# Fewer filler matmuls between the first scores and the first rows: 5 in place of 24

## The chip, the cores and the metric

The kernel runs on one core of one Trainium2 chip. Its time is the device time of one execution in microseconds (us), lower is better. Times in the trace count from the first instruction of the profiled execution.

## The reference, cut to what matters

Three stages follow one another: a blockwise decayed linear attention, a Fourier mixing with a layer norm and a two-layer network, and a second layer norm with another network. The change touches the attention stage only.

```python
def _attn_ref(q, k, v, lam):                 # B, H, S, D = 2, 8, 768, 64
    ...
    for b in range(nb):                      # blocks of tokens
        intra = np.einsum('bhic,bhjc->bhij', qb, kb) * Dmask[None]
        intra = np.einsum('bhij,bhjd->bhid', intra, vb)
        inter = np.einsum('bhid,bhde->bhie', qb * lam_pow[None], kv_state)
        out[:, :, sl] = intra + inter
        kb_dec = kb * rev_pow[None]
        kv_state = lam_block * kv_state + np.einsum('bhsd,bhse->bhde', kb_dec, vb)
    return out

def reference(**kwargs):
    attn_out = _attn_ref(**attn_kwargs)
    x = ...                                  # (2, 768, 512)
    x = _moe_ref(x=x, **moe_kwargs)          # x + Re(FFT2(x)), norm, 512 -> 2048 -> 512
    return _moe2_ref(x=x, **moe2_kwargs)     # norm, 512 -> 2048 -> 512
```

## The kernel before, in words

Every engine has a program of its own, written out by hand, and semaphores tie them together; there is no scheduler. The order of the work on an engine is the order in its program.

The attention stage works in NBLK = 6 blocks of 128 tokens and B = 2 batches, which gives 12 units (block c, batch b). TensorE has three kinds of steps for a unit, all on f32 data:

- **scores** (`scores_of`, line 374): keys times queries, 8 products, each of 64 rows of the array and 128 columns moved. The product for the even head of a pair lies on partitions 0 to 63, that for the odd head on 64 to 127.
- **keys-values** (`keys_values`, line 387): the block's addition to the state, 8 products with outputs of 64 partitions each. It waits for kd, GpSimd's product of line 1314.
- **rows** (`rows`, lines 404 and 409): masked scores times values (line 409, 8 products of 64 columns), and from block 1 on queries times state (line 404, 4 products of 128 columns). It waits for the masks of VectorE (line 924) and, from block 1, for qd (GpSimd, line 1303) and the state.

An f32 product appears as two instructions in the trace, so a full rows step is 8 instructions of line 404 and 16 of line 409, and a scores step is 16 of line 374.

At the start the order on TensorE is: a wait for the first zeroed state tile (GpSimd, line 1289); 11 filler matmuls (line 417, WARM_BEFORE); scores(0, 0) and scores(0, 1); 24 filler matmuls (line 422, WARM_BETWEEN); a wait for the first values (v_first); rows(0, 0), keys-values(0, 0), rows(0, 1), scores(1, 0), keys-values(0, 1). A loop over blocks 1 to 4 follows, in each of which stand scores(c, 1), keys-values(c, 0), rows(c, 0), scores(c+1, 0), keys-values(c, 1), rows(c, 1). At the end come scores(5, 1), rows(5, 0) and rows(5, 1). A filler matmul multiplies a 128x128 f16 tile of zeros by 128x512 zeros into bank 7, which nobody reads; the bank is later the keys-values output of batch 1, written with start=True.

The masks need the decay matrix DT. VectorE makes the powers of lam (line 908), SyncE writes them to pow_dram (line 274) and reads them back as DT (line 278); the copy of line 913 and the first masks (line 924) wait for that. SyncE's queue loads blocks c = 2 to 5 into two alternating buffers: queries and keys (line 261) wait for qk_done and qd_done, keys and values by token (line 264) for pv_done and kv_done, which TensorE counts up. Weight chunks (line 243) are loaded in between.

Behind the attention stage TensorE goes on with the Fourier products `sequence` (line 472), then `features` (line 491), and for the rest of the kernel with the networks (lines 552 and 572). ScalarE copies each rows result out (line 680), and VectorE (lines 956, 957, 985, 986) and GpSimd (lines 1325, 1326) fold these for the Fourier products.

Of the kernel before, what the change touches and what calls it, by code (L numbers as in the profile page):

```python
# [60 lines left out]
S1, S2, S3, S4, A12, A11, A22 = range(7)  # L61
B11, T1, B21, B22, T3, T2, T4 = X_ORDER = range(7)

WARM_BEFORE, WARM_BETWEEN = 11, 24
LATE = {2: 4, 3: 5}


# [1443 lines left out]
```

## Time and profile before

| | us |
|---|---|
| median of 3 executions | 622.82 |
| lowest, highest | 621.06, 626.46 |
| the profiled execution's own time | 626.46 |
| its span, first to last instruction | 624.5 |

The profile is of one execution. PE is TensorE's matmuls, PEld its weight loads, DVE VectorE, ACT ScalarE, POOL GpSimd, SPq SyncE's DMA queue. The ends of matmuls are modelled, so neighbouring groups overlap by some tenths of a us; where lengths are added up, the distance from one start to the next is used. "Granted clock" is the share of TensorE's full 2.4 GHz that the chip let through: 1.00 is 2.4 GHz, 0.50 is 1.2 GHz.

### The profile page before, as it was taken

The numbers are of one execution on the slowest core, as the hardware profiler recorded it, in microseconds if no ns is written. First come the engines' busy times: TensorE is split into PE (matmuls) and PEld (weight loads), VectorE is DVE, ScalarE is ACT, GpSimd is POOL, SyncE is SP. The second block draws the span as 40 slices with busy tenths as digits, with TensorE's granted clock in tenths as the row PEclk, the third lists the DMA queues.
The fourth block names the chain that finished last, engine by engine and source line by source line (L and its number), as shares of the span: only waits on it lengthen the run. The fifth ranks groups of instructions, "written<-read, shape, count | busy, mean of one in ns | idle before, by whom it ended". The sixth has DMA issues, their size and how long they took to land.

```text
span 624.5 us, 10866 instructions
## 1 busy us (share of the span) xinstructions
PE 597.9 (96%) x4143; PEld 407.7 (65%) x4143; DVE 371.2 (59%) x637; ACT 242.4 (39%) x488; POOL 152.7 (24%) x133
## 2 busy tenths in 40 slices
PE   8999899978989999999999999999999999999997
PEld 4898656745666666666666666576666666666664
DVE  2569948967678586556676888733345334433223
ACT  0332143643465432443356675234422344232231
POOL 1547644833532000110322763001000010000000
PEclk9999699979999999999999999999999999999999
DMA  8999780000000263331123231100001000010001
GB/s 243 392 382 382 274 243 1 1 2 1 0 2 1 76 162 102 101 102 44 60 68 99 71 116 54 34 2 1 1 26 44 1 2 1 0 68 1 1 2 68
DMA packets 41412, 50.43 MB, mean 81 GB/s; under 512 B 2442, under 2 KB 28690, under 8 KB 39956
## 3 DMA queue, kind: packets, MB, share of 16 engines
q1 hardware_dynamic: 39156, 45.05, 21.9%
q10 hardware_dynamic: 1728, 3.15, 1.3%
q0 software_dynamic: 480, 1.57, 0.9%
q8 instruction: 32, 0.52, 0.3%
q14 instruction: 16, 0.13, 0.1%
HBM read 43.46 MB, written 6.30 MB: 80 GB/s over the span
## 4 chain that ended last, share of the span: by engine, by line
PE 66%; DVE 11%; POOL 7%; issue 7%; DMA 5%; ACT 3%; SPq 1%; DVEq 0%; ACTq 0%; POOLq 0%
PE bank L572 30%; PE bank L552 26%; PE bank L472 4%; DMA arena<-attn 3%; PE bank L409 2%; DMA arena<-w 1%; PE bank L404 1%; DVE arena L1034 1%; PE bank L541 1%; POOL arena L1410 1%; DVE arena L1042 1%; DVE arena L1035 1%; DVE arena L1155 1%; POOL arena L1357 1%; POOL arena L1354 1%
## 5 line engine op out<-in xcount | busy, mean ns | idle before, releaser
L572 PE MATMUL bank<-arena 128*128 128x512 f16 x1152 | 288.2, 380 | 2.9 <-DVE arena L1163 2.0
L552 PE MATMUL bank<-arena 128*128 128x256 f16 x2016 | 262.6, 275 | 9.6 <-DVE arena L1204 6.7
L552 PEld LDWEIGHTS bank<-arena 128*128 128x128 f16 x2016 | 198.2, 99 | 85.0 <-DVE arena L1204 7.6
L572 PEld LDWEIGHTS bank<-arena 128*128 128x128 f16 x1152 | 112.7, 98 | 90.2 <-DVE arena L1163 2.6
L1155 DVE SCALAR_TENSOR_TENSOR arena<-arena 128x512 f16<-128x512 f32 x96 | 71.1, 741 | 76.4 <-ACT arena L804 76.3
L804 ACT ACTIVATE arena<-arena 128x512 f16<-128x512 f32 x96 | 60.4, 629 | 101.0 <-DVE arena L1204 95.6
L1198 DVE SCALAR_TENSOR_TENSOR arena<-bank,arena 128x256 f32<-128x256 f32 x48 | 20.2, 422 | 71.8 <-PE bank L552 71.8
L1367 POOL TENSOR_TENSOR arena<-arena 128x512 f32<-128x512 f32 x6 | 8.3, 1379 | 150.9 <-ACT arena L775 90.8
L1149 DVE TENSOR_TENSOR arena<-arena 128x512 f16<-128x512 f32 x42 | 35.5, 855 | 12.2 <-ACT arena L788 12.2
L859 ACT ACTIVATE arena<-bank 128x256 f32<-128x256 f32 x48 | 18.3, 382 | 58.2 <-PE bank L552 58.2
L968 DVE TENSOR_REDUCE arena<-arena 128x1 f32<-128x1024 f32 x32 | 38.3, 1209 | 0.0
L1204 DVE SCALAR_TENSOR_TENSOR arena<-bank,arena 128x256 f32<-128x256 f32 x48 | 20.2, 420 | 27.1 <-PE bank L552 27.1
L472 PE MATMUL bank<-arena 128*128 128x385 f32 (+1 forms) x96 | 34.3, 514 | 0.0
L822 ACT ACTIVATE arena<-bank 128x256 f32<-128x256 f32 x48 | 18.4, 383 | 40.2 <-PE bank L552 40.1
L1182 DVE SCALAR_TENSOR_TENSOR arena<-bank,arena 128x256 f32<-128x256 f32 x48 | 20.2, 421 | 20.2 <-PE bank L552 20.2
L1354 POOL TENSOR_TENSOR arena<-arena 128x256 f32<-128x256 f32 x16 | 14.6, 910 | 69.8 <-DMA arena<-w 65.5
L836 ACT ACTIVATE arena<-bank 128x256 f32<-128x256 f32 x48 | 18.3, 382 | 29.1 <-PE bank L552 29.1
L815 ACT ACTIVATE arena<-bank 128x256 f32<-128x256 f32 x48 | 18.1, 377 | 27.5 <-PE bank L552 27.5
L409 PE MATMUL bank<-arena 128*128 128x64 f32 x192 | 27.8, 275 | 0.7 <-DVE arena L924 0.7
L409 PEld LDWEIGHTS bank<-arena 128*128 128x128 f32 x192 | 26.6, 204 | 1.2 <-issue 1.2
L472 PEld LDWEIGHTS bank<-arena 128*128 128x128 f32 x96 | 18.9, 201 | 12.9 <-issue 2.3
L788 ACT ACTIVATE arena<-arena 128x512 f16<-128x512 f32 x42 | 26.1, 624 | 1.5 <-POOL arena L1374 1.3
(97 smaller groups left out, 556.7 us busy)
## 6 DMA issues: line engine op xcount, KB each, us to landing
arena<-w SPq DMA_DIRECT2D x48, 256.0 KB, 4.5
arena<-w SPq DMA_DIRECT2D x24, 512.0 KB, 3.8
arena<-attn SPq DMA_DIRECT2D x10, 1024.0 KB, 8.8
x_dram<-arena ACTq DMA_DIRECT2D x12, 256.0 KB, 6.5
out<-arena SPq DMA_DIRECT2D x12, 256.0 KB, 2.1
arena<-attn SPq DMA_DIRECT2D x4, 512.0 KB, 4.3
arena<-c SPq DMA_DIRECT2D x1, 1153.5 KB, 11.0
arena<-g SPq DMA_DIRECT2D x1, 514.0 KB, 12.6
```

The source lines that it names most:

```text
L409: last = nc.tensor.matmul(xps[b][:, h * D:(h + 1) * D], PT[b][:, par, pair, :], v, start=first, stop=True, skip_group_check=not first)
L472: last = nc.tensor.matmul(f1_bank[f % 3][:, 0:n], lhs, C1[:, c, par * NE:par * NE + n], start=c == 0, stop=c == HALF - 1)
L552: last = nc.tensor.matmul(bank_, wst[:, i, wx, w, kt, :], xs[s % 2][:, ux, x, kt, :], start=not started and k == 0, stop=k == 5, skip_grou ...
L572: last = nc.tensor.matmul(ops[t][:], hT[n % 2][:, half, hx, t * P:(t + 1) * P], wdn[:, i, wx, half * DM:(half + 1) * DM], start=first and ...
L788: nc.scalar.activation(xs[s % 2][:, 0, which, :, :], x_block(which), ACT.Copy).then_inc(xh_done, 1)
L804: nc.scalar.activation(hT[n % 2][:, half, 0, :], z[n % 2][:, half, :], ACT.Relu).then_inc(hh_done, 1)
L968: nc.vector.tensor_reduce(wmax_chunks[:, m, c:c + 1], raw, AX.X, ALU.max, apply_absolute_value=True).then_inc(wred[m], 1)
L1149: nc.vector.tensor_tensor(xs[s % 2][:, 1, which, :, :], x_block(which), xs[s % 2][:, 0, which, :, :], ALU.subtract).then_inc(xl_done, 1)
L1155: nc.vector.scalar_tensor_tensor(hT[n % 2][:, half, 1, :], z[n % 2][:, half, :], 0.0, hT[n % 2][:, half, 0, :], ALU.max, ALU.subtract).the ...
L1182: nc.vector.scalar_tensor_tensor(z[n % 2][:, 0, 0:HT], chain[1 - n % 2], H_SCALE, p1, ALU.mult, ALU.add).then_inc(z11_out, 1)
L1198: nc.vector.scalar_tensor_tensor(z[n % 2][:, 1, 0:HT], seventh[:, 0:HT], H_SCALE, u2, ALU.mult, ALU.add).then_inc(z21_out, 1)
L1354: nc.gpsimd.tensor_tensor(s1, a21, a22, ALU.add).then_inc(ws_step, 1)
```

## The change

The constant WARM_BETWEEN goes from 24 to 5; nothing else changes. The loop of lines 421 and 422 then issues 5 filler matmuls.

```diff
-WARM_BEFORE, WARM_BETWEEN = 11, 24
+WARM_BEFORE, WARM_BETWEEN = 11, 5
```

## Rows read from the trace of the kernel before

**Rows 1.** The page: granted clock in 40 slices of 15.6 us; the chain's shares.

```profile
PEclk9999699979999999999999999999999999999999
...
PE 66%; DVE 11%; POOL 7%; issue 7%; DMA 5%; ACT 3%; SPq 1%; DVEq 0%; ACTq 0%; POOLq 0%
```

**Rows 2.** Timeline of TensorE: start, length, line, count, idle time before and its releaser.

```profile
7.47 5.35 PE L422 MATMUL bank<-arena 128*128 128x512 f16 x24
13.53 1.97 PE L409 MATMUL bank<-arena 128*128 128x64 f32 x16 [0.71 <-DVE arena L924]
16.03 0.69 PE L387 MATMUL bank<-arena 128*64 128x64 f32 x16 [0.52 <-POOL arena L1314]
16.64 2.00 PE L409 MATMUL bank<-arena 128*128 128x64 f32 x16
18.57 1.16 PE L374 MATMUL bank<-arena 64*128 64x128 f32 x16
...
22.15 0.69 PE L387 MATMUL bank<-arena 128*64 128x64 f32 x16 [0.71 <-POOL arena L1314]
...
25.58 1.16 PE L374 MATMUL bank<-arena 64*128 64x128 f32 x16
26.68 0.69 PE L387 MATMUL bank<-arena 128*64 128x64 f32 x16
27.29 0.49 PE L404 MATMUL bank<-arena 128*128 128x128 f32 x2
...
30.11 1.16 PE L374 MATMUL bank<-arena 64*128 64x128 f32 x16
```

**Rows 3.** Timeline of VectorE, around the first masks, and the fold of one unit.

```profile
11.96 0.24 DVE L913 COPY arena<-arena 128x4 f32<-128x4 f32 x2 [8.06 <-DMA arena<-pow_dram]
12.10 2.48 DVE L924 TENSOR_TENSOR arena<-bank,arena 128x512 f32<-128x512 f32 x4
...
60.79 1.46 DVE L956 TENSOR_TENSOR arena<-arena 128x512 f32<-128x512 f32 x1
62.17 1.75 DVE L957 TENSOR_TENSOR arena<-arena 128x512 f32<-128x512 f32 x1
```

**Rows 4.** The chain that ended last, in order of time: start, length, what.

```profile
9.81 7.68 DMA arena<-attn
...
17.63 2.35 POOL arena L1303
...
22.15 0.69 PE bank L387 x16
```

**Rows 5.** Busy time by stretch; after POOL: the granted clock, DMA share, GB/s.

```profile
63.50:65.70 2.20, 0.05 (x1) 0.00 (x0) 2.20 (x4) 0.60 (x1) 2.20 (x2) 1.00 1.05 404
65.70:71.50 5.80, 5.11 (x24) 5.14 (x25) 5.25 (x6) 0.00 (x0) 2.28 (x2) 0.50 0.57 214
71.50:75.90 4.40, 4.40 (x9) 2.50 (x9) 3.49 (x5) 0.76 (x3) 2.11 (x2) 0.50 0.63 195
...
124.70:127.10 2.40, 0.04 (x1) 0.00 (x0) 2.37 (x6) 1.10 (x2) 1.92 (x3) 1.00 0.01 3
129.10:133.90 4.80, 4.80 (x23) 3.44 (x24) 2.37 (x4) 2.95 (x5) 2.07 (x3) 0.50 0.00 0
```

**Rows 6.** Timeline of TensorE, rows(5, 1) and the first Fourier products.

```profile
66.39 0.77 PE L404 MATMUL bank<-arena 128*128 128x128 f32 x2 [2.85 <-DVE arena L924]
...
71.54 10.16 PE L472 MATMUL bank<-arena 128*128 128x385 f32 x24
```

**Rows 7.** Groups by line and form, 0 to 75 us.

```profile
L409 PE MATMUL bank<-arena 128*128 128x64 f32 x192 | 27.8, 275 | 0.7 <-DVE arena L924 0.7
...
L404 PE MATMUL bank<-arena 128*128 128x128 f32 x80 | 19.2, 324 | 3.8 <-DVE arena L924 3.8
```

**Rows 8.** Waits of TensorE, 13 to 75 us: total, times, longest.

```profile
PE bank L404 <- DVE arena L924: 3.8, 2, 2.8
PE bank L387 <- POOL arena L1314: 2.2, 4, 0.7
```

## The prediction

> **What bounds the kernel now.** I read the page first. TensorE gives 66% of the chain that ended last, so it is the engine whose time counts; its granted clock reads 9 or 10 tenths in all but two of the 40 slices [rows 1]. The change sits in the first 14 us, so the rest is read there.
>
> The TensorE timeline of that stretch gives the order of work. The 24 extra matmuls (line 422) run from 7.47 to 12.82 us. TensorE then waits 0.71 us, until 13.53, for the first masks of VectorE (line 924) [rows 2]. Those masks start with VectorE's copy at 11.96, which had waited 8.06 us for the transfer of the decay rows out of pow_dram [rows 3]. The chain of waits agrees: from 9.81 to 22.15 us it holds a load of the attention inputs and GpSimd's products, and no TensorE work. TensorE enters it at 22.15 [rows 4]. So the 24 matmuls hold up nobody. Their results in bank 7 are never read; the first keys-times-values product of batch 1 overwrites that bank.
>
> **What the change removes and adds.** It removes 19 of 24 matmuls and adds nothing: no wait, DMA or buffer. Start to start the 24 take 5.35 us, 0.22 us each; five take 1.1 us. TensorE is then done at about 7.47 + 1.1 = 8.6 us, and the next thing in its queue, rows(0, 0), still waits for the masks. It starts at 13.53 as now. Directly the change gains 0 us. What it makes is an idle stretch of 13.53 - 8.6 = 4.9 us where TensorE now has 0.7.
>
> **What that idle stretch does to the clock.** The table by stretch shows where the granted clock fell from 1.00 to 0.50, from 2.4 to 1.2 GHz. A TensorE idle stretch stands before each fall: 2.2 us from 63.5, clock down at 65.7; 2.4 us from 124.7, clock down at 127.1 [rows 5]. The waits of 0.52 and 0.71 us in the attention stage did not let it fall [rows 2]. A stretch of 4.9 us is twice the longer of those two. I take the fall as nearly certain (95%), some 2 to 4 us into the gap, so that rows(0, 0) starts at 1.2 GHz.
>
> **When it comes back.** This decides the time, and the rows leave it open. Two restarts at 1.2 GHz are the ones to compare:
> - at 129.1, dense f16 matmuls of 256 columns: clock back after 4.8 us;
> - at 66.39, rows(5, 1), small f32 products of 128 and 64 columns: TensorE is busy for 5.15 us without a gap and the clock stays at 0.50. It comes back at 75.9, after 4.4 us of the wide f32 products of line 472 [rows 5, 6].
>
> The attention stage of 13.5 to 71.5 us is made of just what did not bring the clock back. Rows products take 2.82 of each 4.53 us unit (27.29 to 30.11 of 25.58 to 30.11); the rest is scores of 1.10 us on half the array's rows and key-value products of 0.61 us on half its columns [rows 2]. No row shows these two at 1.2 GHz. I take the nearest row, rows(5, 1), and forecast that the clock stays down until line 472.
>
> The Trainium skill (TensorE: Matmul & The Clock Gate, "Why this matters for your kernels") speaks against that: it says that continuous TensorE work gets the clock to full rate. This trace agrees for the restart at 129.1, and does not for 66.39 to 71.54. By that rule alone the time would be about 624.5 us, the third rival's; by the row it is the sum below.
>
> **The sum.** Work of TensorE from 13.53 to 71.54, start to start [rows 2, 6]. The program has 2 first rows steps, and 10 each of full rows, scores and key-value steps; the forms agree (line 404 is there 80 times, 8 a full step; line 409 192 times, 16 for each of 12) [rows 7]:
> - 2 x 1.95 + 10 x 2.82 + 10 x 1.10 + 10 x 0.61: 3.9 + 28.2 + 11.0 + 6.1 = 49.2 us at full clock;
> - waits of 2.2 us for GpSimd (four, line 387) and 3.8 us for VectorE (two, line 404) [rows 8], and 5.15 - 2.82 = 2.3 us because rows(5, 1) ran slow: 57.5, against 58.0 measured.
>
> At 1.2 GHz a full rows step takes 5.15 us, 1.83 times 2.82. With that factor on all: 7.1 + 51.5 + 20.1 + 11.2 = 89.9 us. The six waits go: they are for GpSimd, VectorE and loads, which keep their speed while TensorE takes 8.3 instead of 4.5 us a unit. The attention stage ends at 13.53 + 89.9 = 103.4 instead of 71.54: 31.9 us later.
>
> Nothing behind it takes this back. SyncE's loads wait for TensorE's counts (pv_done, kv_done), so SyncE and GpSimd move with it; VectorE's fold of a unit (1.5 + 1.8 us, lines 956 and 957 [rows 3]) fits in the 5.15 us of rows(5, 1), so line 472 starts at once. It starts at 1.2 GHz in both kernels. Its first step is TensorE's own in the chain, so the delay passes through whole.
>
> Bounds: were scores and key-value products not slowed at all, 7.1 + 51.5 + 11.0 + 6.1 = 75.7 us, so +17.7; were they slowed by the full clock ratio of 2, 7.1 + 51.5 + 22.0 + 12.2 = 92.8, so +34.8. I take 1.83, the one factor that is measured on this stage. The profiled execution took 626.46 us, 3.6 over the median of 622.82, and would come to 658.4; against the median, 622.8 + 31.9 = **655 us**, own range 640 to 659.
>
> **The rivals.**
> 1. *The clock comes back in the scores and key-value products* (chance 0.32). Behind the two first rows stand scores, key-value, scores, key-value without a rows step between them, two instructions side by side on the array's halves, denser than rows. For it: no row shows them failing to bring the clock back. Against it: each fills only half the array, and nothing of this kind is seen to raise the clock. TensorE would reach the end of that scores step at 13.53 + 3.6 + 1.1 + 3.6 + 2.0 + 1.1 + 2.0 = 26.9 us, where it now starts the next product at 22.15: 4.8 us late; with an earlier return 3.9. The later waits, 3.8 + 2.2 - 0.52 - 0.71 = 4.8 us less the 2.85 before rows(5, 1), can take back up to 1.9. That leaves 2 to 4.8 us, taken as 4: 627 us. The 2.85 us are behind VectorE's folds, which move with TensorE.
> 2. *It comes back late, in the middle of the stage* (0.10), where scores and key-value products happen to fall together. Each unit run slow costs 8.3 - 4.5 = 3.8 us; two to six units on top of the first rival give 634 to 650.
> 3. *Any 5 us of work brings it back* (0.08). 5 us at 1.83 lose 2.3 us, of which the waits of 0.52 and 0.71 us cover 1.2: 624.5 us. The row at 66.39 speaks against it.
> 4. *The clock doesn't fall* (0.03): the change is free, 623 us.
> 5. *Faster* (0.02). The removed matmuls are in the way after all: where the pow_dram transfer lands early, the masks are ready before 12.82 and rows(0, 0) is held by the 24. The price is at most 12.82 - 8.6 = 4.2 us, and it counts from the point where the masks are over 0.7 us early, if the clock also stays up. Against it: the chain up to 22.15 doesn't contain TensorE, so an earlier rows(0, 0) has nothing to bring forward: 622 us.
>
> **How the numbers follow.** The forecast has 0.45. About 1% is what a measurement of this kernel can tell from no change: 6.2 us. Slower by more: the forecast, rival 2, and the upper end of rival 1 (0.05), 0.60. Within it: the rest of rival 1 and rivals 3 and 4, 0.38. Faster by more: 0.02, since even rival 5 hardly reaches it. The range runs from 623.5, which takes in rivals 1 to 3, to 659, the forecast's upper end.
>
> **What would show it.** Right: no line-422 matmul after about 8.7 us; the granted clock at 0.50 before 14.5; rows steps of 5.15 us and units of some 8.3 throughout; line 472 starting near 103; after it the same stages with the same lengths. Rival 1 shows as a clock of 1.00 from 25 to 29 us and line 472 starting near 76. Wrong altogether would be a clock at 1.00 from 8.6 on, or a stage end moved by other than TensorE's slow time.

## The result and the profile after

The change costs a little: 626.69 us (625.41 to 631.13) against 624.45 (621.06 to 626.46), 14 executions each. The ratio is 1.0051, interval 1.0034 to 1.0068. The forecast was 655, 32 us over before; what came is 2.2 us by the medians, 3.2 by the ratio. Rival 1 stood at 627. The ratios in this text leave out five executions that stand far above the others of their kernel: 631, 631 and 1034 us of before, 2011 us without fillers and 639.7 us with 14.

The TensorE timeline after, from the first rows on (start, length, line, count, idle time before), answers to [rows 2]:

```profile
13.75 3.65 PE L409 MATMUL bank<-arena 128*128 128x64 f32 x16 [4.90 <-DVE arena L924]
17.33 1.12 PE L387 MATMUL bank<-arena 128*64 128x64 f32 x16
18.38 3.68 PE L409 MATMUL bank<-arena 128*128 128x64 f32 x16
21.99 2.08 PE L374 MATMUL bank<-arena 64*128 64x128 f32 x16
24.00 1.12 PE L387 MATMUL bank<-arena 128*64 128x64 f32 x16
25.05 1.23 PE L374 MATMUL bank<-arena 64*128 64x128 f32 x16
26.21 0.69 PE L387 MATMUL bank<-arena 128*64 128x64 f32 x16
```

The idle stretch is 4.90 us, as worked out. The first rows take 3.6 us a step in place of 1.95. Then the second scores step takes 1.23 us, not 2.08: the clock came back inside it. The table by stretch (TensorE's busy time first; the granted clock stands behind the GpSimd columns) says the same, and is to be read against [rows 5]:

```profile
8.70:11.50 2.80, 0.15 (x1) 0.00 (x0) 0.00 (x0) 0.00 (x0) 0.00 (x0) 1.00 0.88 216
11.60:13.70 2.10, 0.00 (x0) 0.00 (x0) 1.52 (x5) 0.00 (x0) 0.00 (x0) 0.50 1.08 271
13.70:22.00 8.30, 8.25 (x50) 7.92 (x50) 1.52 (x3) 1.43 (x3) 5.42 (x3) 0.50 1.02 385
22.00:25.20 3.20, 3.20 (x35) 2.86 (x34) 1.08 (x2) 0.60 (x1) 0.75 (x1) 0.50 0.84 285
25.30:29.20 3.90, 3.90 (x53) 3.71 (x54) 3.90 (x6) 0.83 (x2) 2.32 (x1) 1.00 0.77 229
```

The key-value product that started at 22.15 before starts at 26.21: 4.1 us late. Then the kernel catches up twice. Inside the attention stage, the waits of TensorE for GpSimd (2.2 us in [rows 8]) are all gone. The wait for VectorE before the rows step at 60.69, 0.99 us before the change, is 1.32 us now; that step starts at 63.93, 3.2 us late. In this pair of profiles the rest is given back behind the stage, as the starts of the same groups show. Before:

```profile
92.63 2.05 PE L491 MATMUL bank<-arena 128*128 128x129 f32 x16
...
129.06 5.17 PE L552 MATMUL bank<-arena 128*128 128x256 f16 x24 [4.32 <-DVE arena L1204]
154.29 1.36 PE L552 MATMUL bank<-arena 128*128 128x256 f16 x6 [2.36 <-DVE arena L1204]
172.70 1.47 PE L552 MATMUL bank<-arena 128*128 128x256 f16 x12 [1.52 <-issue]
```

After:

```profile
69.63 0.77 PE L404 MATMUL bank<-arena 128*128 128x128 f32 x2 [2.84 <-DVE arena L924]
74.78 8.80 PE L472 MATMUL bank<-arena 128*128 128x385 f32 x24
...
94.51 2.05 PE L491 MATMUL bank<-arena 128*128 128x129 f32 x16
...
130.96 4.46 PE L552 MATMUL bank<-arena 128*128 128x256 f16 x24 [4.33 <-DVE arena L1204]
155.50 0.83 PE L552 MATMUL bank<-arena 128*128 128x256 f16 x6 [2.37 <-DVE arena L1204]
172.62 1.47 PE L552 MATMUL bank<-arena 128*128 128x256 f16 x12 [1.65 <-issue]
```

The lag is 74.78 - 71.54 = 3.2 us at line 472, 1.9 at lines 491 and 552, 1.2 at the wait before 155 and -0.1 at 172.6. It shrinks just where the clock is slow before the change and less so after it. The first 24 instructions of line 472 take 8.80 us and not 10.16 [rows 6], since the slow clock leaves them after 1.6 us and not 4.4. The product at 129 takes 4.46 and not 5.17. The one at 154 runs at full clock. The stretches behind the stage:

```profile
74.80:76.40 1.60, 1.60 (x4) 0.98 (x4) 0.75 (x2) 0.60 (x1) 0.00 (x0) 0.50 0.21 41
131.00:134.40 3.40, 3.40 (x17) 2.44 (x18) 1.59 (x2) 2.52 (x4) 2.07 (x3) 0.51 0.00 0
```

So this execution after ran at 0.50 for 13.7 us at the start (11.6 to 25.2) and had less slow time later: 10.2 us behind the stage's last wait (69.6 to 76.4 and 131.0 to 134.4) where before has 20.5 (65.7 to 75.9, 127.1 to 133.9 and 154.4 to 157.8). Its span of 624.2 us against 624.5 is not the whole story: the medians are 2.2 us apart, and "The change by itself" below shows that most executions differ from this pair.

### The profile page after: what moved, and what is told of

Same layout as the page of the kernel before. It is cut to its first block, busy times and chain, and to the rows that moved or that the text cites. A ratio compares the mean times of both kernels' runs of the same rounds, so it can differ in the third digit from the quotient of the medians.

```text
span 624.2 us, 10828 instructions
## 1 busy us (share of the span) xinstructions
PE 595.3 (95%) x4124; PEld 409.2 (66%) x4124; DVE 371.4 (60%) x637; ACT 242.6 (39%) x488; POOL 151.9 (24%) x133
## 4 chain that ended last, share of the span: by engine, by line
PE 70%; DVE 13%; issue 7%; POOL 5%; ACT 3%; DMA 2%; SPq 0%; DVEq 0%; ACTq 0%; POOLq 0%
PE bank L572 30%; PE bank L552 26%; PE bank L472 4%; PE bank L409 3%; PE bank L404 2%; PE bank L374 2%; DVE arena L1034 1%; DVE arena L1042 1%; DVE arena L1155 1%; DVE arena L1035 1%; PE bank L541 1%; POOL arena L1410 1%; DVE arena L1149 1%; PE bank L387 1%; DVE arena L1163 1%
## 5 line engine op out<-in xcount | busy, mean ns | idle before, releaser
L1204 DVE SCALAR_TENSOR_TENSOR arena<-bank,arena 128x256 f32<-128x256 f32 x48 | 20.1, 420 | 27.1 <-PE bank L552 27.1
L409 PE MATMUL bank<-arena 128*128 128x64 f32 x192 | 31.2, 300 | 4.9 <-DVE arena L924 4.9
L409 PEld LDWEIGHTS bank<-arena 128*128 128x128 f32 x192 | 29.8, 227 | 5.5 <-issue 5.4
L472 PE MATMUL bank<-arena 128*128 128x385 f32 (+1 forms) x96 | 32.9, 498 | 0.0
L472 PEld LDWEIGHTS bank<-arena 128*128 128x128 f32 x96 | 18.3, 195 | 12.1 <-issue 0.8
```

Of the source, the lines that this page charges most:

```text
L409: last = nc.tensor.matmul(xps[b][:, h * D:(h + 1) * D], PT[b][:, par, pair, :], v, start=first, stop=True, skip_group_check=not first)
L472: last = nc.tensor.matmul(f1_bank[f % 3][:, 0:n], lhs, C1[:, c, par * NE:par * NE + n], start=c == 0, stop=c == HALF - 1)
L1204: nc.vector.scalar_tensor_tensor(z[n % 2][:, 1, HT:TOK], a, H_SCALE, p7, ALU.mult, ALU.add).then_inc(z22_out, 1)
```

## The experiments

In the profiles of kernels with added lines the line numbers behind the addition are some higher; 475 there is 472 here, 555 is 552.

**Which work brings the clock back.** Three kernels, each the kernel after with one addition, put extra work of one kind before rows(0, 0), where TensorE restarts at 1.2 GHz. Its results are not used. Each ran once.

```diff
             pe.wait_ge(v_first, 16)
+            pe.wait_ge(mask_done, 2)
+            for _ in range(3):
+                for h in range(H):
+                    pair, par = divmod(h, 2)
+                    nc.tensor.matmul(bank[6][:, h * D:(h + 1) * D], PT[0][:, par, pair, :],
+                                     blk_in[0][:, 3, pair, D * par:D * par + D], start=True, stop=True)
             rows(0, 0, 0, True)
```

> The kernel after, with three more steps of the kind of rows(0, 0) (line-409 products of 64 columns, 8 a step, into bank 6) right behind the first masks; their results are not used. Theory A (the kind of work decides: rows steps do not raise the clock, scores and key-value steps do): the clock is still at 0.50 through all three extra steps and the two first rows steps, 5 x 3.6 us and one key-value step of 1.1, and comes back only in the scores and key-value steps behind, at about 34 to 38 us. Theory B (any continuous work of 11 to 12 us raises it, as after 13.75 us in the kernel after): the clock is back at about 25 us, in the middle of the extra rows.

Measured: 636.94 us in one execution, 622.38 for before beside it. The table by stretch of extra_rows:

```profile
13.50:23.80 10.30, 10.23 (x48) 10.26 (x49) 1.12 (x2) 0.00 (x0) 6.16 (x3) 0.50 0.96 343
23.80:32.00 8.20, 8.20 (x50) 7.89 (x49) 0.42 (x1) 1.43 (x3) 0.00 (x0) 0.50 0.10 35
32.10:35.60 3.50, 3.50 (x37) 3.16 (x38) 1.43 (x3) 0.60 (x1) 0.28 (x1) 0.50 0.20 75
35.70:40.00 4.30, 4.30 (x56) 4.04 (x56) 4.12 (x6) 0.86 (x3) 1.98 (x1) 1.00 0.84 259
```

From 13.57 to 32.0 us TensorE works without a gap on rows steps, with one key-value step among them, and the clock stays at 0.50. Then come scores and key-values, and it is up 3.6 us later. Theory B falls: under it the clock would have been back at about 25 us.

For the scores kind the loop is:

```diff
+            for _ in range(5):
+                for pair in range(PAIRS):
+                    for par in range(2):
+                        r = slice(64 * par, 64 * par + 64)
+                        nc.tensor.matmul(bank[6 + par][:, pair * P:(pair + 1) * P], PT[0][r, 0, pair, :],
+                                         PT[0][r, 1, pair, :], start=True, stop=True)
```

> The kernel after, with five more steps of the kind of scores (f32 products of 64 rows and 128 columns, two side by side, into banks 6 and 7) right behind the first masks, on masked scores as data; results not used. Theory A: the clock is back 3 to 7 us after the restart, at 17 to 21 us, so that rows(0, 0) runs at 0.12 us an instruction and not 0.23. Theory B: back at about 25 us, after all five extra steps at 2.1 us each.

For the key-value kind it is:

```diff
+            pe.wait_ge(kd_done, 1)
+            for _ in range(9):
+                for h in range(H):
+                    pair, par = divmod(h, 2)
+                    nc.tensor.matmul(bank[6][D * par:D * par + D, pair * D:(pair + 1) * D], kd[0][:, h, :],
+                                     blk_in[0][:, 3, pair, D * par:D * par + D], start=True, stop=True)
```

> The kernel after, with nine more steps of the kind of keys-values (f32 products of 64 columns with 64 output partitions, two side by side, into bank 6) behind the first key product of GpSimd, so from about 16 us; results not used. Theory A with key-value steps as effective as scores: the clock is back 3 to 7 us after 16.5, at 20 to 24 us. Theory A with scores alone effective: still 0.50 until the scores behind rows(0, 1), at 30 us or later. Theory B: back at about 28 us, with the nine steps over at 26.

Measured: 629.88 and 633.34 us. The stretches of extra_scores:

```profile
14.30:18.40 4.10, 4.04 (x38) 4.07 (x40) 1.11 (x2) 0.00 (x0) 2.13 (x2) 0.50 1.01 408
18.50:21.00 2.50, 2.50 (x47) 2.38 (x43) 0.00 (x0) 0.00 (x0) 2.36 (x2) 1.00 0.99 402
```

And of extra_keys_values:

```profile
15.70:21.20 5.50, 5.44 (x102) 5.47 (x104) 0.00 (x0) 0.00 (x0) 3.80 (x2) 0.50 1.00 409
21.30:22.50 1.20, 1.20 (x46) 1.20 (x42) 0.00 (x0) 0.00 (x0) 0.37 (x1) 1.00 1.05 293
```

Scores alone bring the clock back after 4.1 us, key-values alone after 5.5. Each fills half the array only, and does it all the same. The first rows after them run at full clock (2.00 us a step). The kinds of step differ in several ways at once: in the size of the products, in the part of the array they fill and in whether two lie side by side. The runs show which kinds raise the clock, not which of these properties does it.

**Are the late falls chance?** Two kernels were run again as they were.

> The kernel after as it is, for a second profile. Both theories: clock down between 11 and 14 us, back between 24 and 29 us, line 472 starting 2 to 5 us later than the 71.54 of before. If the later falls of the clock are set by chance, their number and places differ from the first profile while the attention stage's end does not by more than 1 to 2 us.

> The kernel before as it is, for a second profile. The clock stays at 1.00 from the first scores to the wait before rows(5, 1), line 472 starts at 71 to 72 us. If the later falls are set by chance, they differ from the first profile (20.5 us at 0.50 in three places).

Measured: after 624.72 us, clock down at 11.4 and back at 25.1, line 472 at 74.26; before 625.83 us, line 472 at 71.19. The lag is 3.1 us, the first pair's 3.2. The later falls came in the same places as in the first profiles, some tenths of a us apart: 64.9, 126.4 and 153.7 before; 69.4 and 130.9 after. These four profiles show two patterns, one for each kernel. They don't show that every execution follows them: the mean clocks of the other executions, below, differ.

**How many fillers it takes.**

```diff
-WARM_BEFORE, WARM_BETWEEN = 11, 24
+WARM_BEFORE, WARM_BETWEEN = 11, 0
```

> No filler matmul between scores(0, 1) and rows(0, 0). TensorE idle from 7.5 to 13.6 us, so the clock falls as in the kernel after or one step sooner, and the rest is the same: with theory A the same time as the kernel after, 0.3 to 0.7% above before. If instead each removed filler had its own price, it would be at 0.6% or more, growing with the gap.

The ratio is 1.0053 (1.0032 to 1.0075): five fillers and none are alike. With 14 and with 19 in that place:

> 14 filler matmuls, over at about 10.5 us, idle for 3 us before rows(0, 0), less than the 4.9 of the kernel after and just over the 2.2 and 2.4 us after which the clock fell elsewhere. Theory A: the clock falls in some executions and not in others, ratio to before between 1.000 and 1.005; where it falls, the attention stage ends 2 to 4 us later, where not, as before.

> 19 filler matmuls, over at about 11.7 us, idle for 1.8 us before rows(0, 0). The waits of 0.99 and under left the clock up, 2.2 us let it fall. Theory A: between the two; 1.8 us and thin rows behind it let it stay up in most executions, ratio 0.998 to 1.003; a clock that falls behind the wait of GpSimd at 16 us, as with 14 fillers, would show that the thin rows count as little as idleness.

With 14 the ratio is 1.0055 (1.0028 to 1.0083); in its profile the idle time was 2.0 us and not 3, rows(0, 0) ran at full clock, and the clock fell behind another idle time of 0.9 us, at 16.4, and was back at 26.6. That it falls in some executions and not in others isn't borne out for 14: none has a mean clock above 0.986, where before's reaches 0.994. With 19 it is 1.0007 (0.9971 to 1.0044), and that mean hides two groups: four executions at 620.9 to 622.4 us with a mean clock of 0.992 to 0.994, six at 626.2 to 628.0 with 0.981 to 0.984. The profiled one is of the second group:

```profile
14.18 2.58 PE L409 MATMUL bank<-arena 128*128 128x64 f32 x16 [2.27 <-DVE arena L924]
16.69 1.12 PE L387 MATMUL bank<-arena 128*64 128x64 f32 x16
```

Here the idle time was 2.27 us, longer than the 1.8 worked out, and the clock fell at 15.4, inside rows(0, 0). So the expectation for 19, that it stays up in most executions, failed: the idle time was longer than worked out, since the masks came later. By the mean clocks there are executions of both kinds; which of them kept the clock up at the start was not profiled. Of the counts tried, only the 24 that reach up to the masks held it up in every profile.

**Filling the later waits.** The kernel before (24 fillers) with work in the wait before rows(5, 1):

```diff
             rows(last_block, 0, 1, False)
+            pe.wait_ge(ex_done, UNITS - B)
+            for _ in range(3):
+                nc.tensor.matmul(bank[7][:], DT[:, 0, 0, :], DT[:, 0, :, :], start=True, stop=True)
             rows(last_block, 1, 1, False)
```

> The kernel before with 3 f32 matmuls of 128x512 (0.86 us each, results not used) in the wait of 2.85 us before rows(5, 1), line 404. If an idle stretch alone brings the clock down and it is the slow clock from 65.7 to 75.9 that costs, the clock stays at 1.00 there, rows(5, 1) takes 2.8 us and not 5.15, the first 4.4 us of line 472 take some 2.2: 4.5 us less in all, ratio 0.993. If the stage behind is bound by loads or VectorE, the attention stage ends 2.3 us sooner but the total does not move.

Measured: ratio 0.9991 (0.9970 to 1.0012). The clock and the steps came as expected; the groups of line 404 and 475 in its timeline:

```profile
66.26 0.46 PE L404 MATMUL bank<-arena 128*128 128x128 f32 x2 [0.21 <-DVE arena L927]
...
69.27 8.00 PE L475 MATMUL bank<-arena 128*128 128x385 f32 x24
```

Line 472 starts 2.3 us sooner and its first group takes 8.00 us, not 10.16; the profiled span is 620.1 us. The median is down by 0.8 us only. So the expectation of 0.993 missed for the kernel as a whole, and why the other executions gain less than the profiled one was not settled by this run. What the list of executions shows is that before's own time goes with its mean clock: 620.35 to 621.86 us at 0.991 to 0.994, and 624.52 to 626.00 at 0.984 to 0.989. From the mean clock the slow time can be estimated: twice what it lacks of 1.00, times the span. For the profiled execution of before that gives 20.0 us, and its table by stretch has 20.5. The median over the 55 executions of before in this round and the next is 13.7 us, over the 12 of fill_late 9.3. So most executions of before have less slow time than the two profiled ones, and there is less to win in them: 4.4 us of slow time, not 10.2. That is an argument, not a test.

Then a second wait was filled too, the one of 4.3 us at 125 to 129 us:

```diff
+                if n == 0:
+                    pe.wait_ge(de_done, HALF)
+                for _ in range(32 if n == 0 else 0):
+                    nc.tensor.matmul(bank[5][:, 0:HT], wst[:, 0, 0, 0, 0, :], xs[0][:, 0, 0, 0, :],
+                                     start=True, stop=True)
                 pe.wait_ge(z22_out, n + 1)
                 product(n, a, S4, B22, True, p3_done)
```

> fill_late with 32 more f16 matmuls of 256 columns (0.11 us each at full clock, results not used, into bank 5) in the wait of 4.3 us before the line-552 product at 129 us. If the clock falls only for want of TensorE work, it stays up there too, the product that took 4.8 us at 0.50 takes 2.6, and the whole gains 2 us on fill_late; against before the ratio is 0.993 to 0.997. If the fillers merely shift work, it equals fill_late, 0.999.

Measured: 619.62 us (617.85 to 623.02), ratio 0.9946 (0.9921 to 0.9971). Its interval lies wholly below 1, which neither fill_late's nor after's does. The product that took 5.17 us takes 2.82:

```profile
124.25 2.82 PE L555 MATMUL bank<-arena 128*128 128x256 f16 x24 [0.83 <-DVE arena L1212]
```

**The change by itself.** The same kernel with 5 fillers for 24:

> fill_all with WARM_BETWEEN = 5, so the change under study on a kernel whose later waits do not let the clock fall. If the small price of the change (0.5%) is the delay of the attention stage less what the first 10 us of line 472 give back because their slow stretch is shorter, then here, where line 472 is not slow, nothing is given back: line 472 starts 3 us later than in fill_all, and the whole is 3 us slower, 0.5% above fill_all by medians. If the loads or VectorE had absorbed part of the delay behind the stage, it would be 2 us or less here too.

Measured: 624.32 us (622.16 to 625.32), ratio to before 1.0007 (0.9984 to 1.0030). Against fill_all that is 4.7 us by the medians, and 1.0007 / 0.9946 = 1.0061, 3.8 us, by the ratios. The timeline of fill_all:

```profile
21.93 0.69 PE L387 MATMUL bank<-arena 128*64 128x64 f32 x16 [0.73 <-POOL arena L1322]
...
68.88 8.00 PE L475 MATMUL bank<-arena 128*128 128x385 f32 x24
```

And of fill_all_5:

```profile
27.13 0.69 PE L387 MATMUL bank<-arena 128*64 128x64 f32 x16
...
73.64 6.71 PE L475 MATMUL bank<-arena 128*128 128x385 f32 x20
```

The key-value product is 5.2 us late, line 472 is 4.8 us late, and the span is 622.1 against 617.2: 4.9 us, the lag at line 472 within 0.2. Nothing is given back behind the stage. That was the expectation. Its size was 3 us, and the lag is 1.6 us more than the 3.2 of the kernel under study: 1.1 us of that is there at the key-value product already (5.2 against 4.1 us), since the clock in this execution came back at 27.1 and not 25.2. Loads and VectorE absorb nothing behind the stage.

In the first pair of profiles the shorter slow time behind the stage gave 3 us back. In most executions it does not, by the estimate from the mean clock. The median of after's 14 is 27.5 us of slow time, that of before 13.7. Four profiles (after, after_again, between_0, fill_all_5) have 13.7 us of it at the start; taken off, 13.8 us are left behind the stage in after, as much as in before. Executions with equal slow time there can be set side by side: with 10.2 us, 15 of before have a median of 623.0 us and 5 of after 625.6; with 13.7 us, 11 of before 624.4 and 5 of after 627.5. That is 2.6 and 3.1 us, near the lag of 3.2 us at line 472 and the 3.2 us of the ratio. So the small price is the lag of the attention stage itself, and the equal spans of the first pair are a matter of which executions were profiled. This is worked out from mean clocks, partly of other rounds; no profile of such an execution of before exists.

## Why the prediction was wrong

- **The fillers hold up nobody, the gain is 0**: right. rows(0, 0) starts at 13.75 us, 13.53 before, released by the masks in both.
- **The idle stretch of 4.9 us and the fall**: right, 4.90 us, and the clock fell at 11.6.
- **When it comes back**: this step failed. The clock came back at 25.2 us and not at line 472, so the stage ends 3.2 us late and not 31.9. The prediction took rows(5, 1) as the row nearest to scores and key-values, because those fill only half the array, and gave the whole stage that row's behaviour. extra_rows shows the row itself read rightly: 18 us of nearly nothing but rows leave the clock down. extra_scores and extra_keys_values show that it does not carry over: they raise it in 4.1 and 5.5 us. What I should have weighed more is that no row showed scores or key-values failing to raise the clock; the prediction says so in rival 1, names their two instructions side by side, and gives it 0.32. Whether lying side by side is the reason, no run shows.
- **The factor of 1.83**: about right where it applied. Start to start, scores take 2.01 against 1.10 us (1.83), key-values 1.05 against 0.61 (1.72), first rows 3.6 against 1.95 (1.85).
- **Nothing behind takes it back**: right in the filled kernel (4.8 us late at line 472, 4.9 at the end), and by the mean clocks in most executions of this one. In the first pair of profiles it did not hold: line 472 and the products at 129 and 154 us were themselves slow before, and less so after. "It starts at 1.2 GHz in both kernels" was true, and said nothing of how long.
- **Rival 1**: its mechanism is what happened. It had 26.9 us for the product that came at 26.21, 4.8 us late against 4.1 measured (5.2 in fill_all_5), since the clock came back within the second scores step. That its 627 us meets 626.69 is partly luck: it stands on a median of 622.82 from three executions, where 14 give 624.45, so its 4 us were 2.2 to 3.2.
- **Rival 3**: its sum was off. 622.8 us and the 1.1 us that its own terms leave make 623.9, not 624.5. extra_rows rules its mechanism out.
- **The Trainium skill's rule** (TensorE: Matmul & The Clock Gate, "Why this matters for your kernels"), that continuous TensorE work gets the full clock: the runs bear it out for scores, key-values, wide f32 and f16 products, and not for rows steps. In extra_rows TensorE was busy in 10.23 of 10.30 us and went on so to 32 us at 0.50.

What stays open: which property of a step decides whether it raises the clock; and why the change costs 3.8 to 4.7 us in the filled kernel and 2.2 to 3.2 here. The later return of the clock accounts for 1.1 us in the profiled executions, and whether it comes that late in most executions of fill_all_5 is not known.

## What to carry to other kernels

Filler matmuls that cost nothing on the path can still be worth their place: look at the TensorE idle time that appears when they go, and compare it with those idle stretches of the same trace after which the clock fell. To price a fall, find the first work behind it that is seen to raise the clock; a busy engine is not enough, as 18 us of small products at 1.2 GHz show here. Look also at what was slow already, and at more than one execution: two profiles can differ in their slow time by as much as the change costs. Filling two such waits was worth 0.5% here, where one alone gave nothing clear of noise.

## What was not expected of the hardware

- The clock stayed at 0.50 through 18 us of unbroken f32 products of 64 columns, each with its own weight load, but rose after 4.1 us of products on 64 rows and after 5.5 us of products on 64 output partitions.
- At full clock the same thin rows keep it: from 25.3 us on in the kernel after, units with 2.8 us of rows in 4.5 ran to the wait before rows(5, 1) at 1.00. Each of these units also has 1.7 us of scores and key-values, so this does not show that rows alone would keep it up.
- The clock fell in rows(0, 0), while TensorE was working, 1.2 us behind an idle stretch of 2.27 us (19 fillers). In the same kernel four of ten executions have a mean clock of 0.992 to 0.994 against its 0.981.
